# Attention stage of a fused kernel: key loads in four pieces, summary rows written by VectorE, the 1/8 scale in the mask add, expert 0 on ScalarE's queue, x transposes ahead of weighing

## What is computed

```python
# attention: B, H, S, D = 2, 8, 768, 64; block, window = 32, 16
k_sum = k.reshape(B, H, nb, block, D).max(axis=3)
v_sum = v.reshape(B, H, nb, block, D).mean(axis=3)
scores_l = scale * (q @ k.T), masked to |i - j| < window      # scale = 1/8
scores_s = scale * (q @ k_sum.T) + log(block)
a = softmax(concat(scores_l, scores_s)); x = a @ concat(v, v_sum)
# experts: E, F = 8, 1024
logits = x @ w_gate; e = argmax(logits), or the token before's where sigmoid(x @ w_local) >= 0.5
out = softmax(logits)[e] * (relu(x @ w1[e]) @ w2[e])
# mixing
theta = x @ w_theta; zr, zi = x * cos(theta), x * sin(theta)
u = x + w_tok_r @ zr + w_tok_i @ zi; out = u + relu(u @ w_ch)
```

## Time and profile before

| what | value |
|---|---|
| timed runs, us | 474.62, 476.86, 477.51 (median 476.86) |
| the profiled execution, us | 477.65 |
| its span, first to last instruction, us | 475.7 |
| mean granted TensorE clock | 0.964 |
| busy: PE, DVE, ACT, POOL, us | 426.8, 245.6, 188.7, 54.6 |
| end of the attention stage (last of L1038), us from the start | about 84.1 |

### The profile page before, as it was taken

The page is one execution under the profiler, slowest core; times in us unless marked ns, Lnnn a source line. Parts: engine busy times, 40 slices in busy tenths (PEclk is TensorE's granted clock), DMA queues, the critical chain, the costliest instruction groups (busy, mean ns, idle before and its releaser), DMA issues.

```text
span 475.7 us, 8142 instructions
## 1 busy us (share of the span) xinstructions
PE 426.8 (90%) x2800; PEld 340.4 (72%) x2801; DVE 245.6 (52%) x395; ACT 188.7 (40%) x425; POOL 54.6 (11%) x96
## 2 busy tenths in 40 slices
PE   8588887238999999999999896999999999999987
PEld 3477776116888888888888644788887778888875
DVE  3687894679124563226521304666657655456253
ACT  1766895026335363346522423433333321322020
POOL 3223421014000010000100044000000000000000
PEclk9998999559999999999999998999999999999999
DMA  8989693821951116410111246000000000000112
GB/s 333 303 273 334 223 328 102 347 72 32 360 228 45 44 44 256 184 32 35 43 45 33 101 123 251 0 1 0 1 1 0 1 22 23 22 23 0 44 45 88
DMA packets 12909, 52.90 MB, mean 111 GB/s; under 512 B 1745, under 2 KB 1873, under 8 KB 11345
## 3 DMA queue, kind: packets, MB, share of 16 engines
q1 hardware_dynamic: 7584, 37.57, 21.5%
q0 software_dynamic: 3424, 11.54, 7.5%
q10 hardware_dynamic: 1872, 3.41, 1.9%
HBM read 61.95 MB, written 11.53 MB: 154 GB/s over the span
## 4 chain that ended last, share of the span: by engine, by line
PE 74%; DVE 12%; ACT 5%; DMA 4%; issue 3%; ACTq 0%; POOL 0%; SPq 0%; DVEq 0%; POOLq 0%
PE ps L1112 15%; PE ps L1114 14%; PE ps L1113 14%; PE ps L1224 6%; PE ps L1222 6%; PE ps L1223 6%; PE ps L1015 3%; PE ps L1187 2%; PE ps L1136 2%; ACT p L525 2%; DMA v<-v_win 2%; DMA kfull<-k_full 1%; PE ps L1000 1%; PE ps L1024 1%; PE ps L1119 1%
## 5 line engine op out<-in xcount | busy, mean ns | idle before, releaser
L1222 PE MATMUL ps<-z_h,mix_h 128*128 128x512 f32 x144 | 57.2, 397 | 0.0
L1224 PE MATMUL ps<-z_h,mix_l 128*128 128x512 f32 x144 | 56.2, 390 | 0.0
L1223 PE MATMUL ps<-z_l,mix_h 128*128 128x512 f32 x144 | 56.0, 389 | 0.0
L1112 PE MATMUL ps<-w_h,hT_h 128*128 128x512 f32 x104 | 42.5, 408 | 1.8 <-DVE hT_l L863 1.8
L1112 PE MATMUL ps<-w_h,xT_h 128*128 128x512 f32 x104 | 41.6, 400 | 1.0 <-DVE xT_l L857 1.0
L525 ACT ACTIVATE p<-s,bias 128x120 f32<-128x120 f32 x96 | 36.5, 383 | 12.1 <-DVE bias L699 11.9
L1113 PE MATMUL ps<-w_h,hT_l 128*128 128x512 f32 x104 | 41.2, 396 | 0.0
L1114 PE MATMUL ps<-w_l,hT_h 128*128 128x512 f32 x104 | 41.2, 396 | 0.0
L1114 PE MATMUL ps<-w_l,xT_h 128*128 128x512 f32 x104 | 40.8, 392 | 0.0
L1113 PE MATMUL ps<-w_h,xT_l 128*128 128x512 f32 x104 | 40.7, 391 | 0.0
L863 DVE TENSOR_TENSOR hT_l<-ps,hT_h 128x512 fp32r<-128x512 f32 x26 | 16.7, 686 | 46.0 <-ACT hT_h L588 46.0
(11 more groups left out here) (182 smaller groups left out, 853.3 us busy)
## 6 DMA issues: line engine op xcount, KB each, us to landing
w_raw<-w SPq DMA_DIRECT2D x16, 2048.0 KB
v<-v_win SPq DMA_DIRECT2D x24, 192.0 KB, 4.5
mix_raw<-mix SPq DMA_DIRECT2D x1, 4608.0 KB, 14.0
ys<-y_sb ACTq DMA_DIRECT2D x13, 256.0 KB
kfull<-k_full SPq DMA_DIRECT2D x4, 800.0 KB, 10.8
vfull_sb<-v_full SPq DMA_DIRECT2D x2, 1536.0 KB, 11.8
xd<-x_sb POOLq DMA_DIRECT2D x12, 256.0 KB, 4.1
out<-o SPq DMA_DIRECT2D x12, 256.0 KB, 2.0
```

The costliest lines, as they stand in the source:

```text
L1112: pe.matmul(ps[:, bank, :], a_h[:, k, :], w_h[:, n, :], start=(k == 0), stop=False)
L1222: pe.matmul(ps[:, t, :], w_h, zh, start=(jb == 0 and m == 0), stop=False)
L1223: pe.matmul(ps[:, t, :], w_h, zl, start=False, stop=False)
L1224: mm = pe.matmul(ps[:, t, :], w_l, zh, start=False, stop=(jb == TPB - 1 and m == 1))
```

## The change

It has six parts.

1. The keys of a batch are loaded in four transfers, one for each pair (128 x 800 numbers, 400 KB), each with a semaphore of its own, and VectorE takes the block maxima pair by pair (four instructions with 24 results a partition in place of two with 48). Those of batch 1 stand behind tile 1 (one), tile 2 (two) and tile 3 (one).
2. The scores get 128 columns a head in PSUM in place of 120, and `s` is seen as eight heads of 120.
3. One `scalar_tensor_tensor` multiplies the scores by 1/8 and adds a mask that isn't scaled any more. ScalarE takes exp(s + nmax); `bias` and its instruction and semaphore are gone.
4. For tile 0 VectorE writes the value summaries to `v` itself, by eight copies of 24 x 128 from PSUM, ahead of its tile 0. ScalarE's `vsum_copy(0)` waits for them, and GpSimd only writes the rows of tile 1's buffer.
5. w1 and w2 of expert 0 are issued from ScalarE, behind its tiles 3 and 6.
6. On TensorE `transpose_x(g-1)` stands ahead of `weigh(g)`.

```diff
-    mask = np.full((P, 3, NK), MASKED * math.sqrt(D), np.float32)
+    mask = np.full((P, 3, NK), MASKED, np.float32)
...
-        mask[:, m][summary] = math.log(BLOCK) * math.sqrt(D)
+        mask[:, m][summary] = math.log(BLOCK)
...
-        s_ps = ps[:, B_SC:B_SC + 2, 0:PAIRS * NK].rearrange("p a (b k) -> p a b k", k=NK)
+        s_ps = ps[:, B_SC:B_SC + 2, :].rearrange("p a (b k) -> p (a b) k", k=P)[:, :, 0:NK]
...
             def load_keys(b):
-                for a in range(2):
-                    pairs = slice(a * PAIRS // 2, (a + 1) * PAIRS // 2)
-                    sp.dma_start(kfull_sb[b][:, pairs, :], kfull_d[b, :, pairs, :]).then_inc(kfull_in[b][a], 16)
+                for a in range(PAIRS):
+                    sp.dma_start(kfull_sb[b][:, a, :], kfull_d[b, :, a, :]).then_inc(kfull_in[b][a], 16)
...
-                if g == NT - 7:
-                    sp.dma_start(w1_raw[:, :, :], w1_d[0]).then_inc(w1_in, 16)
-                if g == NT - 4:
-                    sp.dma_start(w2_raw[:, :, :], w2_d[0]).then_inc(w2_in, 16)
...
                 for a in range(2):
+                    pairs = slice(a * PAIRS // 2, (a + 1) * PAIRS // 2)
                     if g in (0, TPB):
-                        pool.wait_ge(kfull_in[b][a], 16)
-                    pairs = slice(a * PAIRS // 2, (a + 1) * PAIRS // 2)
+                        pool.wait_ge(kfull_in[b][pairs.start], 16)
+                        pool.wait_ge(kfull_in[b][pairs.start + 1], 16)
...
-                pool.wait_ge(kmax_done, 2 * (b + 1))
+                pool.wait_ge(kmax_done, PAIRS * (b + 1))
...
-                pool.wait_ge(rows_set, 2 * b + s + 1)
+                pool.wait_ge(rows_set, 2 * b + s)
...
-            for s in range(2):
-                value_rows(0, s, 4)
+            value_rows(0, 1, 4)
...
-                if b:
-                    act.wait_ge(vsum_set[1], b)
+                act.wait_ge(vsum_set[b], 1)
...
-                    act.wait_ge(bias_ready, g + 1)
+                    act.wait_ge(nmax_done, g + 1)
...
-                    e = act.activation(p_sb[s][:, n // PAIRS, n % PAIRS, :], s_sb[s][:, n // PAIRS, n % PAIRS, :], ACT.Exp,
-                                       bias=bias[s][:, n:n + 1], scale=1.0 / math.sqrt(D), accum_out=rsum[s][:, n:n + 1])
+                    e = act.activation(p_sb[s][:, n // PAIRS, n % PAIRS, :], s_sb[s][:, n, :], ACT.Exp,
+                                       bias=nmax[s][:, n:n + 1], accum_out=rsum[s][:, n:n + 1])
...
                 tile(g, g % 2, ex=g + 1 < NT)
+                if g == 3:
+                    act.dma_start(w1_raw[:, :, :], w1_d[0]).then_inc(w1_in, 16)
+                if g == TPB:
+                    act.dma_start(w2_raw[:, :, :], w2_d[0]).then_inc(w2_in, 16)
...
-                    dve.tensor_reduce(out=kmax[:, b * PAIRS + half.start:b * PAIRS + half.stop, :],
-                                      in_=kfull_sb[b][:, half, WINDOW:WINDOW + S].rearrange("p a (n k) -> p a n k", k=BLOCK),
+                    dve.tensor_reduce(out=kmax[:, b * PAIRS + a, :],
+                                      in_=kfull_sb[b][:, a, WINDOW:WINDOW + S].rearrange("p (n k) -> p n k", k=BLOCK),
                                       op=ALU.max, axis=AX).then_inc(kmax_done, 1)
...
-                dve.tensor_tensor(s_sb[s][:, :, :, :], s_ps, masks[:, edge.get(g % TPB, 1), :].unsqueeze(1).unsqueeze(1).broadcast_to([P, 2, PAIRS, NK]),
-                                  ALU.add).then_inc(scores_taken, 1)
+                dve.scalar_tensor_tensor(s_sb[s][:, :, :], s_ps, 1.0 / math.sqrt(D),
+                                         masks[:, edge.get(g % TPB, 1), :].unsqueeze(1).broadcast_to([P, H, NK]),
+                                         ALU.mult, ALU.add).then_inc(scores_taken, 1)
...
-                dve.wait_ge(nmax_done, g + 1)
-                dve.tensor_scalar(bias[s][:, :], nmax[s][:, :], 1.0 / math.sqrt(D), None, ALU.mult).then_inc(bias_ready, 1)
...
+            dve.wait_ge(vsum_ready, 1)
+            for u in range(2):
+                for c in range(KD):
+                    e = dve.tensor_copy(v_sb[0][WK * u:WK * u + NB, u, c * P:(c + 1) * P], ps[CG * c:CG * c + NB, B_VSUM, 0:P])
+            e.then_inc(vsum_set[0], 1)
             for g in range(NT):
                 tile(g, g % 2)
-                if 1 <= g < 3:
-                    key_summary(1, [g - 1])
+                key_summary(1, {1: [0], 2: [1, 2], 3: [3]}.get(g, []))
...
-                weigh(g, s, rounds, b, first)
                 if xt:
                     transpose_x(g - 1, xt_first)
+                weigh(g, s, rounds, b, first)
```

More of the change, by code:

```diff
@@ L209, in program @@
         kmax = sb("kmax", [P, B * PAIRS, NB])
-        s_sb = [sb(f"s{s}", [P, 2, PAIRS, NK]) for s in range(2)]
+        s_sb = [sb(f"s{s}", [P, H, NK]) for s in range(2)]
         p_sb = [sb(f"p{s}", [P, 2, PAIRS, NK]) for s in range(2)]
         nmax = [sb(f"nmax{s}", [P, H]) for s in range(2)]
-        bias = [sb(f"bias{s}", [P, H]) for s in range(2)]
         rsum = [sb(f"rsum{s}", [P, H]) for s in range(2)]
@@ L261, in program @@
         const_in, rconst_in, wg_in = sem("const_in"), sem("rconst_in"), sem("wg_in")
-        kfull_in, vfull_in = [[sem(f"kfull_in{b}{a}") for a in range(2)] for b in range(B)], sem("vfull_in")
+        kfull_in, vfull_in = [[sem(f"kfull_in{b}{a}") for a in range(PAIRS)] for b in range(B)], sem("vfull_in")
         q_in = [sem(f"q_in{n}") for n in range(4)]
@@ L269, in program @@
         scores_ready, scores_taken = sem("scores_ready"), sem("scores_taken")
-        nmax_done, bias_ready, exp_done = sem("nmax_done"), sem("bias_ready"), sem("exp_done")
+        nmax_done, exp_done = sem("nmax_done"), sem("exp_done")
         pT_ready, pT_even, pT_odd = sem("pT_ready"), sem("pT_even"), sem("pT_odd")
@@ L675, in _, with key_summary @@
             iota = const[:, C_IOTA:C_SCAN].rearrange("p (j e) -> p j e", e=E)
-            def key_summary(b, halves=range(2)):
-                for a in halves:
-                    half = slice(a * PAIRS // 2, (a + 1) * PAIRS // 2)
+            def key_summary(b, pairs):
+                for a in pairs:
                     dve.wait_ge(kfull_in[b][a], 16)
-                    dve.tensor_reduce(out=kmax[:, b * PAIRS + half.start:b * PAIRS + half.stop, :],
-                                      in_=kfull_sb[b][:, half, WINDOW:WINDOW + S].rearrange("p a (n k) -> p a n k", k=BLOCK),
+                    dve.tensor_reduce(out=kmax[:, b * PAIRS + a, :],
+                                      in_=kfull_sb[b][:, a, WINDOW:WINDOW + S].rearrange("p (n k) -> p n k", k=BLOCK),
                                       op=ALU.max, axis=AX).then_inc(kmax_done, 1)
@@ L692, in scores @@
                     dve.wait_ge(exp_done, g - 1)
-                dve.tensor_tensor(s_sb[s][:, :, :, :], s_ps, masks[:, edge.get(g % TPB, 1), :].unsqueeze(1).unsqueeze(1).broadcast_to([P, 2, PAIRS, NK]),
-                                  ALU.add).then_inc(scores_taken, 1)
+                dve.scalar_tensor_tensor(s_sb[s][:, :, :], s_ps, 1.0 / math.sqrt(D),
+                                         masks[:, edge.get(g % TPB, 1), :].unsqueeze(1).broadcast_to([P, H, NK]),
+                                         ALU.mult, ALU.add).then_inc(scores_taken, 1)
                 dve.wait_ge(scores_taken, g + 1)
-                dve.tensor_reduce(out=nmax[s][:, :], in_=s_sb[s][:, :, :, :].rearrange("p a b k -> p (a b) k"),
+                dve.tensor_reduce(out=nmax[s][:, :], in_=s_sb[s][:, :, :],
                                   op=ALU.max, axis=AX, negate=True).then_inc(nmax_done, 1)
-                dve.wait_ge(nmax_done, g + 1)
-                dve.tensor_scalar(bias[s][:, :], nmax[s][:, :], 1.0 / math.sqrt(D), None, ALU.mult).then_inc(bias_ready, 1)
             def pT_copy(g):
@@ L733, in _ @@
             dve.memset(half_pi[:, :], math.pi / 2).then_inc(hp_done, 1)
-            key_summary(0)
+            key_summary(0, range(PAIRS))
             dve.wait_ge(const_in, 16)
@@ L989, in scores @@
                             at = u * (NB + SUB)
-                            mm = pe.matmul(s_ps[SUB * u:SUB * u + SUB, h, p, :], q_all[rows, g, p, SUB * u:SUB * u + SUB],
+                            mm = pe.matmul(s_ps[SUB * u:SUB * u + SUB, h * PAIRS + p, :], q_all[rows, g, p, SUB * u:SUB * u + SUB],
                                            kw_sb[s][rows, p, at:at + NK], start=True, stop=True)
```

## The result

The changed kernel takes 478.92 us (median of 20 runs, 476.82 to 483.41) where the kernel before takes 475.23 (20 runs, 474.28 to 477.51): the ratio is **1.0079, 95% interval 1.0057 to 1.0101**. Forecast were 470.0 and a range of 467.5 to 474.0. So it is slower by 0.8%, and the prediction has the wrong sign.

The account below looks back on a forecast made before the run. In the first 84 us no engine is full, so waits between engines bound the kernel. T4 -3.5, T4 to T11 -2.5 and the end -0.9 sum to -6.9 us, giving 470.0, likeliest 468.8 to 471.8, 8 in 10 467.5 to 474.0.

Parts of the forecast that it names:

- W0: Tile 0's weighing on TensorE: can start at 21.1 us, not 22.29.
- T4: Tile 4's transposes of p on TensorE: at 38.9 to 39.7 us, not 43.58; -3.5 with 0.8 for the clock.
- T4 to T11: From tile 4's to tile 11's transposes of p: 30.4 us, not 32.89; -2.5.
- With w2 in ScalarE's queue it would share instead of queue: Tile 9's value window, queued behind w2, took 7.79 us, usually 4.5; 0.2 to 0.3 lost at its weighing.
- rival 2: Loads set the middle: w1 beside `vfull` at half rate, T4 at 41 or 42, about 472 us; chance 0.15.
- The start: First tiles: exponentials 0.44 + 0.17 us earlier, at 13.13; W0 at 21.1, not 22.29.
- N1: Tile 1's norm on VectorE: at 26.5 us with full clock, 27.9 if it falls, 29.36 before.
- `vfull` of batch 1: Load for the second value summary: issued 1.2 to 2 us earlier, landing at 37.2 to 38, not about 39.2.
- Tile 9's window: Value window that tile 9's weighing awaited until 70.23, its turn being 70.04: 0.2 to 0.3 us lost.
- rival 4: VectorE's new mask add pays two passes, 1.16 us more: +4.5, about 481 us; chance 0.04.
- loop C: Steady tiles: transposes of p wait for all eight exponentials; 8.76 us for two tiles, 4.38 a tile, not 4.57.
- the end: Last transposes of x wait only for tile 11's norm: 0.69 + 0.04 us after 79.75, not 1.59; -0.9.

Follow-up runs that it names:

- e9: Changed kernel with w1, w2 on SP in 512 KB pieces and `vfull` of batch 1 issued right after the first value summary: 472.91 us, ratio 0.9898.
- e5: Changed kernel with w1, w2 back on SP and the keys loaded in two transfers, not four: 474.71 us, ratio 1.0003.
- e3: Changed kernel with w1, w2 each split into two transfers of 2 KB pieces, still in ScalarE's queue: 474.01 us, ratio 0.9976.
- e8: Changed kernel with w1, w2 back on SP and the transposes of x behind the weighing again: 475.87 us, ratio 1.0012.
- e12: Changed kernel with w1, w2 each split into two transfers of 8 KB pieces, still in ScalarE's queue: 485.11 us, ratio 1.0130.

## Why the prediction was wrong

By its own steps, against the changed kernel and against e1, the change without its moved loads:

| step | predicted | after | e1 | e9 |
|---|---|---|---|---|
| W0 | 21.1 | 22.11 | 22.13 | 22.20 |
| T4 | 38.9 to 39.7, or 1.3 more if the clock falls (0.8 in the sum) | 42.55 | 40.99 | 40.52 |
| T4 to T11 (before 32.89) | 30.4 | 39.23 | 32.84 | 30.39 |
| T11 to the end of the stage (before 7.6) | 6.7 | 6.6 | 6.7 | 6.8 |
| stage over | 77.2 | 88.4 | 80.5 | 77.7 |

- **The step that failed is "With w2 in ScalarE's queue it would share instead of queue"**, with "0.2 to 0.3 lost" today as all that depended on it. It costed a window beside w2 at the usual 4.5 or a little over, and no window beside w1 at all; rival 2 looked at w1 beside `vfull` only, at half rate for 2 us. Measured, tile 4's window took 15.6 (9.3 before) and tile 8's 9.9: while both queues were at work they shared by pieces and not by bytes, and w1's pieces were eight times as long. T4 to T11 is 8.8 us longer than forecast in the changed kernel and 2.4 in e1, so 6.4 of the 8.8 are this part's. The earlier trace rows had the clue, a window that took 7.79 behind w2; I read it as a fault of the queue, when the queue order was what kept all other windows ahead of the weights. The rule that I quoted from the Trainium skill ("DMA: Bandwidth & Descriptors", "Issuing engines are not separate DMA queues") says that another issuing engine saves only issue time. I used it only for `vfull`.
- **The start was mis-sized.** "The last of four key pieces leaves one maximum of some 0.9 behind it, not 1.74" held for the maximum (0.95), but the piece itself landed 0.6 later, against "nothing lands later", and TensorE's constants held it 0.3 longer: -0.44 became 0. The copies cost 0.30 and not 0.20 to 0.283, started 0.7 late with `vfull`, and their reader was ScalarE, whom I had not priced: W0 -0.2 and not -1.2. N1 was at 29.13 (29.36 before, 26.5 to 27.9 forecast). The clock fell there as in the earlier trace rows. In e5, where it didn't, N1 was at 27.59.
- **`vfull` of batch 1** was to land at 37.2 to 38 because it would be issued 1.2 to 2 us earlier. It was issued at 29.32, not at all earlier than before (29.05), and landed at 39.8. e5 issued it 1.2 earlier and got nothing for it. Today's landing, from which it was reckoned, was misread too: the earlier trace rows give 11.8 us for both of its loads, so 40.85 and not 39.2. That the bytes ahead of it set the landing fits these runs and e9, where it went ahead of them and landed at 29.6. That T4 waits for it was right, and that the clock may fall with it too: in the changed kernel, in e3 to e8 and in e12 the summary ran in 2.0 to 2.8 us, not 1.51.
- **Tile 9's window** was costed at 0.2 to 0.3. As TensorE came earlier, it grew: in e1 its wait was 1.69, and transposes at 1.2 GHz followed. With the loads in small pieces (e9) the stretch is as forecast, though the agreement to 0.01 is luck: T4 to T5 took 4.28 and not 4.1, the rest 26.11 and not 26.3.
- **Right:** the mask add at 1.16 (rival 4 is out), loop C (8.67 against 8.76), no key wait at tile 6, and the end (-0.9 against -1.0).

The rivals had a loss of 4.5 us at 0.04, through an addition that turned out to cost nothing. The real loss came through the one part that I had costed as a small gain and given no rival of its own sign.

## What to carry to other kernels

A small transfer with a deadline has its protection from the order within one queue: before moving a large load to another engine's queue, list each small transfer that will be in flight beside it and, where the large load's pieces are fewer than those of the small one's queue, price it as if it landed behind the large one. An earlier issue brought nothing here while the DMA engines were full; a place ahead of the other bytes did. And when waits are taken out of a loop, look for the loads that were just in time: the gain can stop at the first of them (e1 0.5%, e9 1.0%, with the same engine work; the stage over at 80.5 and 77.7).
